# Wider dummy matmuls, a second fold on VectorE in the pairs that issue weights, and one gather moved up

## The reference

```python
batch, n_heads, seq, head_dim = (4, 8, 768, 64)      # chunk = 32, top_k = 6
ub = sum(maximum(q * k_min[chunk], q * k_max[chunk]), -1)   # causal chunks only
sel = the 6 chunks of largest ub, for each query
scores = where(sel & causal, q @ k.T / sqrt(64), -1e9)
attn = exp(scores - max) / (sum(exp(scores - max)) + 1e-09)
x = (attn @ v), heads side by side                   # 3072 tokens x 512
logits = x @ w_gate                                  # 8 experts
expert_idx, gate_w = argmax(logits), its softmax weight
for e in range(8):
    tok_idx = tokens of expert e, the 80 of largest gate_w if there are more
    h = maximum(x[tok_idx] @ w1[e], 0.0)             # 512 -> 1024
    out[tok_idx] = gate_w[tok_idx] * (h @ w2[e])     # 1024 -> 512
```

## Time and profile before

| | us |
|---|---|
| median of 3 runs | 274.03 (273.4 to 276.74) |
| the profiled execution | 270.66 |
| its span, first to last instruction | 268.9 |
| TensorE busy | 258.0 (96%) |
| POOL busy | 216.9 (81%) |
| VectorE busy | 214.0 (80%) |
| ScalarE busy | 149.6 (56%) |

### The profile page before, as it was taken

How to read it: one execution, slowest core, us unless ns; L and a number is a source line. 1 busy time by engine, 2 the same in 40 slices (tenths; PEclk the granted TensorE clock), 3 DMA queues, 4 the chain that set the end, 5 groups by cost and what they waited for, 6 DMA issues and landing times.

```text
span 268.9 us, 9115 instructions
## 1 busy us (share of the span) xinstructions
PE 258.0 (96%) x3812; PEld 164.1 (61%) x3812; DVE 214.0 (80%) x576; ACT 149.6 (56%) x227; POOL 216.9 (81%) x286
## 2 busy tenths in 40 slices
PE   7999999999999999999999999999999998989993
PEld 7456666665656566666655666656565656676663
DVE  6896797687979989777979898999899997983332
ACT  2295656565676564646674546564856564863220
POOL 6067989998999899997999899989999961726862
PEclk9999999999999999999999999999999999999999
DMA  9989999999799979998999899999899896841882
GB/s 149 181 146 151 243 228 275 203 178 224 117 214 170 205 127 195 164 218 142 202 153 214 156 189 157 216 165 311 168 214 258 224 212 161 135 102 39 142 169 77
DMA packets 148616, 48.34 MB, mean 180 GB/s; under 512 B 131583, under 2 KB 138870, under 8 KB 148512
## 3 DMA queue, kind: packets, MB, share of 16 engines
q1 hardware_dynamic: 135504, 28.73, 53.4%
q0 software_dynamic: 9936, 18.64, 38.3%
q10 hardware_dynamic: 3136, 0.39, 0.9%
HBM read 57.03 MB, written 11.01 MB: 253 GB/s over the span
## 4 chain that ended last, share of the span: by engine, by line
PE 62%; POOL 25%; issue 4%; DMA 3%; DVE 3%; ACT 2%; ACTq 1%; POOLq 0%; DVEq 0%
PE OB L632 19%; PE SC L546 19%; POOL ES L600 16%; PE SC L567 4%; POOL EXB L586 4%; PE MM L668 3%; PE MM L474 2%; PE MM L645 2%; PE OB L716 2%; PE OB L1380 2%; DMA qn<-x_rows,idx 1%; DMA qn<-in_q_dram 1%; ACT EXB L576 1%; PE SC L1354 1%; PE MM L513 1%
## 5 line engine op out<-in xcount | busy, mean ns | idle before, releaser
L576 ACT ACTIVATE EXB<-SC 128x1024 f32<-128x1024 f32 (+1 forms) x87 | 83.1, 966 | 36.6 <-PE SC L546 25.0
L600 POOL TENSOR_TENSOR ES<-ES,EXB 128x256 f32<-128x256 f32 (+1 forms) x87 | 91.1, 1048 | 5.6
L546 PE MATMUL SC<-qT,kT 64*128 64x512 f32 (+3 forms) x476 | 86.3, 464 | 0.4 <-ACT EXB L576 0.3
L632 PE MATMUL OB<-EXB,vn 128*64 128x256 f32 (+3 forms) x704 | 73.4, 362 | 0.9 <-POOL EXB L586 0.9
L632 PEld LDWEIGHTS OB<-EXB,vn 128*64 128x64 f32 x704 | 45.9, 137 | 25.7 <-issue 10.4
L546 PEld LDWEIGHTS SC<-qT,kT 64*128 64x128 f32 x476 | 39.2, 187 | 16.5 <-issue 11.0
L600 POOL TENSOR_TENSOR ES<-EXB 128x512 f32<-128x512 f32 (+1 forms) x29 | 45.2, 1559 | 2.4
L586 POOL TENSOR_SCALAR_AFFINE_SELECT EXB<-EXB 128x256 f32<-128x256 f32 x79 | 34.2, 442 | 5.5 <-ACT EXB L576 5.5
L640 ACT ACTIVATE oT<-OB 128x512 f32<-128x512 f32 (+1 forms) x32 | 15.7, 490 | 40.6 <-PE OB L632 40.6
L567 PE MATMUL SC<-unsT,ind 64*128 64x256 bf16 (+5 forms) x238 | 35.6, 295 | 0.1
L567 PEld LDWEIGHTS SC<-unsT,ind 64*128 64x128 bf16 x238 | 11.8, 95 | 15.9 <-issue 6.2
(11 more groups left out here) (269 smaller groups left out, 405.8 us busy)
## 6 DMA issues: line engine op xcount, KB each, us to landing
w1s<-in_moe_w_dram POOLq DMA_DIRECT2D x8, 1024.0 KB, 8.9
w2s<-in_moe_w_dram POOLq DMA_DIRECT2D x7, 1024.0 KB, 13.9
vn<-in_v_dram SPq DMA_DIRECT2D x32, 192.0 KB, 4.4
kn<-in_k_dram SPq DMA_DIRECT2D x62, 96.0 KB, 2.9
qn<-in_q_dram SPq DMA_DIRECT2D x62, 96.0 KB, 3.8
out_dram<-w1s SPq DMA_DIRECT2D x2, 1536.0 KB, 7.0
out_dram<-out_dram SPq DMA_DIRECT2D x2, 1536.0 KB, 9.5
x_rows<-xp SPq DMA_DIRECT2D x7, 384.0 KB, 4.9
```

What stands on the lines that cost most here:

```text
L546: op("pe", lambda: pe.matmul(o, kT[j][pr, ts(kt)], qT[j][pr, q0:q1], start=not flags and (not cols or cols[0] == 0), stop=bool(flags)), r= ...
L576: op("act", lambda: ac.activation(Ex(st, None, 0, W), src, ACTF.Exp, scale=SCALE), r=pk, w=[f"E{st}"])
L600: op(e, lambda: sy.queue[e].tensor_tensor(o, in0, in1, ALU.add), r=[f"E{s2}", f"E{first[0]}"] if first else [f"E{s2}"] + kt, w=kt)
L632: op("pe", lambda: pe.matmul(OB[pr, q0:q1], vn[s][:, kt, h, :], ex, start=(n == 0), stop=last), r=[f"vn{s}{h}", "ES0" if st is None else f ...
```

## The change

1. `warm` issues wide matmuls: one weight load of the identity and up to 4 x 128 columns, the identity read again and again through an access pattern of stride 0. `warm(62)` becomes 15 matmuls of 512 columns and one of 256.
2. `WPLAN` moves ahead of `fold`. In its pairs POOL leaves out (5, 0, 640, 768), and `own_fold` does it on VectorE behind its first addition, on E5 and ES5. Pair 13 is direct and is as before.
3. `turn_next(2)` issues gather 6 behind gathers 4 and 5 and no blocks; `turn_next(3)` issues blocks 0 and 1, `turn_next(4)` gather 7 and blocks 2 and 3, `turn_next(5)` blocks 4 to 7. POOL's order becomes gathers 4, 5 and 6, scatter 0, blocks 0 and 1, scatter 1, gather 7, blocks 2 and 3, blocks 4 to 7, scatter 2.

```diff
+                WPLAN = {2: (0, 1), 4: (2, 3), 6: (4, 5), 8: (6, 7), 10: (8, 9), 12: (10, 11), 13: (12,)}
...
-                    for (s2, c2, q0, q1) in [a for a in ADDS[st] if i in (0, NP - 1) or a != (4, 0, 384, 512) and not (direct(i) and a == (5, 0, 640, 768))]:
+                    for (s2, c2, q0, q1) in [a for a in ADDS[st] if i in (0, NP - 1) or a != (4, 0, 384, 512) and not ((direct(i) or i in WPLAN) and a == (5, 0, 640, 768))]:
...
                         op("dve", lambda: ve.tensor_tensor(o, o, Ex(4, None, 0, 128), ALU.add), r=["E4", "ES3"], w=["ES3"])
+                        if i in WPLAN:
+                            o5 = ES[:, :, 640:768]
+                            op("dve", lambda: ve.tensor_tensor(o5, o5, Ex(5, None, 0, 128), ALU.add), r=["E5", "ES5"], w=["ES5"])
...
                 def warm(n):
-                    for _ in range(n):
-                        op("pe", lambda: pe.matmul(SC[0][:, 0:128], ident_bf[:], ident_bf[:], start=True, stop=True),
+                    for k in range(0, n, 4):
+                        w = min(4, n - k)
+                        op("pe", lambda: pe.matmul(SC[0][:, 0:w * 128], ident_bf[:], bass.AP(ident_bf, 0, [[128, 128], [0, w], [1, 128]]), start=True, stop=True),
                            r=["ident_bf"], w=["SC0"], inc=False)
...
                     if e < 5:
-                        for n in {2: (4, 5), 3: (6,), 4: (7,)}[e]:
+                        for n in {2: (4, 5, 6), 3: (), 4: (7,)}[e]:
                             gather(n, (f"xS{e}",))
-                        last_w2(((0, 1), (2, 3), range(FB // 2, FB))[e - 2])
+                    if 2 < e < 6:
+                        last_w2(((0, 1), (2, 3), range(FB // 2, FB))[e - 3])
```

More of the change, by code:

```diff
@@ L1123, in rank_late @@
                     gate_gcols(bb)
-                WPLAN = {2: (0, 1), 4: (2, 3), 6: (4, 5), 8: (6, 7), 10: (8, 9), 12: (10, 11), 13: (12,)}
                 for i in range(NP):
```

## The result

On the same occasions the kernel before took 273.17 us (median of 22 runs) and the changed kernel 270.42 (median of 22, 269.8 to 273.32): ratio 0.9926, 95% interval 0.9901 to 0.9951, so about 2.0 us by the ratio, where 4.0 were forecast. Ratios here leave out disturbed runs, and the medians do not; so a ratio is not the quotient of the medians beside it.

A forecast was written before the change was run, and what follows sets the result against it. TensorE, busy 258.0 of 268.9 us, bounds the kernel, so only its waits can pay. Gains of 1.0 (part 1), 2.4 (part 2) and 0.65 (part 3) sum to 4.0, taking 274.03 to 270.0 us; range 268.8 to 272.8.

The forecast's parts named there:

- the head: Start of kernel: wide dummies end near 8.0 to 8.5 us, covered by VectorE's work until L474 at 8.63; price 0.
- the hole: Last pair's summing matmuls (L707): a 1.0 us gap from an emptied instruction buffer closes with 92 fewer instructions; gain 1.0.
- Rival 4: Start: the clock rises later, so the first real matmuls run at 1.2 GHz; slower, price taken as 275 us, chance 0.05.
- Rival 1: Last pair's sums (L707): the gap without a releaser stays or moves, so 1.0 us is lost; 271.0 us, chance 0.22.
- what closes counts whole: Behind L707: VectorE waits there and its chain leads to the last gate, so the full 1.0 us is gained.
- Four stretches: Pairs 3, 4, 5 and 9: TensorE's excess over like stretches without weights goes: 0.34, 0.31, 0.88, 0.88, together 2.4 us.
- Rivals 2 and 3: Second fold takes 1.06 us: 272.0 us, chance 0.15; POOL not the cause of TensorE's waits: 272.4 us, chance 0.06.
- rival 2's mechanism: At the second fold, VectorE and POOL get in each other's way, as in POOL's 1.33 against 0.73 us.
- the 0.65: Expert 6's transposes (L1335): gather 6 starts 2.5 us earlier, so TensorE's wait for it goes; gain 0.65 us.
- Gather 7: Expert stage: it arrives at 257.6 where TensorE wants it at about 257.5; loss 0, at worst 0.1 us.
- The blocks that part 3 moves: Expert stage: blocks 0 to 3 move back under 3 us, the last four stay; first used in the last round.
- signs of error: Wrong if L668 waits for the new fold, a new releaserless hole opens, or the first pair's matmuls take twice their time.

The follow-up runs named there:

- e_after2: The changed kernel unaltered, run a third time, on the third chip: 268.03 us, ratio 0.9910 to the kernel before, span 266.2.
- first profile: The first profiled execution of the changed kernel: 270.01 us, span 268.3, against 270.66 and 268.9 for the kernel before.
- e_no3b: Parts 1 and 2 without part 3, run once more on the third chip: 268.91 us, ratio 0.9917 to the kernel before, span 266.2.
- e_pad: The changed kernel plus 46 tiny matmuls behind the wide dummies, restoring TensorE's old instruction count: 269.0 us, ratio 0.9938 to the kernel before.
- e_part1: The kernel before with only part 1, the wide dummies: 269.94 us, ratio 0.9972 to the kernel before.
- e_part2: The kernel before with only part 2, the second fold on VectorE: 267.42 us, ratio 0.9893 to the kernel before.
- e_part3: The kernel before with only part 3, the new order in the expert stage: 271.28 us, ratio 1.0017 to the kernel before.
- e_no1: Parts 2 and 3 with the 62 narrow dummies kept: 274.7 us, ratio 0.9927 to the kernel before.
- e_part2b: Part 2 alone on the kernel before, run once more on the second chip: 273.23 us, ratio 0.9856 to the kernel before.
- e_after: The changed kernel unaltered, run again on the second chip: 273.5 us, ratio 0.9942 to the kernel before, span 271.5.
- e_no3: Parts 1 and 2 without part 3, on the second chip: 270.9 us, ratio 0.9838 to the kernel before.
- e_late_w1: Parts 1 and 2, with the last expert's 1 MB weight block issued behind gathers 2 and 3: 273.19 us, ratio 1.0086 to the kernel before.

## Why the prediction came out as it did

The predicted 270.0 was met by the median of 270.42, partly by luck: the kernel before was at 273.17, not 274.03, on those occasions, and the gain was 1.6 to 2.5 us by the three ratios (0.9942, 0.9926, 0.9910), not 4.0. The execution that answers the sum best is `e_after2`, which has no late copies. Start times of four rows, and the span:

| | before | first profile | `e_after2` | `e_no3b` |
|---|---|---|---|---|
| L645/L650, pair 2 | 38.73 | 38.86 | 38.90 | 38.74 |
| L645/L650, pair 15 | 219.42 | 217.01 | 217.62 | 217.63 |
| L810/L815 | 231.22 | 227.62 | 228.23 | 228.23 |
| first L1354/L1358 | 241.27 | 237.67 | 238.69 | 238.67 |
| span | 268.9 | 268.3 | 266.2 | 266.2 |

Read from `e_after2`: 0.17 lost at the head, 1.97 gained over the pairs, 1.19 at the hole, 0.41 lost at gather 0, 0.12 gained in the expert stage: 2.7 us.

- **Part 1, the head:** right in what counts. VectorE releases L474 in every profile but `e_pad`, at 8.65 to 9.28 us with the wide dummies and 8.60 to 9.01 with the narrow ones, so no price of them shows. The dummies ended at 6.88 to 8.21, mostly earlier than the 8.0 to 8.5 of the prediction: 512 columns take 0.43 us at first and 0.22 later (1.2 and 2.4 GHz), and this step up comes at about 5 us in the first profile and 7.5 in `e_part1`, always ahead of L474. (The granted clock in the earlier trace rows reads 1.00 throughout; the step is read from these distances alone.) Rival 4 is out: L474 and the first scores last as long as before.
- **Part 1, the hole:** the reading held; that a buffer runs empty there is still inferred, but the place is shown. The hole is there in the seven profiles where TensorE has the old number of instructions (both of before, `e_part2`, `e_part3`, `e_pad`, `e_no1`, `e_part2b`; 0.43 to 1.21 us) and at neither place in the seven with 92 fewer. Counted in the trace with its semaphore instructions, TensorE has the same 6,336 or 6,337 instructions ahead of it in all seven. With part 2 there are six semaphore instructions fewer, and the hole stands three matmuls and three weight loads further on, at L727. Rival 1 is out. The Trainium skill (Runtime: NRT & Kernel Launch, Instruction fetch mechanics) calls the crossing of a block boundary mostly hidden; in this run of 128 matmuls and 128 weight loads in 2.6 us the traces disagree.
- **Part 1, what the hole is worth:** the step that failed is "what closes counts whole". Up to L810/L815 it holds: from the last L645/L650 to there it is 10.6 us in all seven profiles without the hole and 11.8 before. Behind that stands gather 0, which waits for the 1 MB block. The issue of the block is released by L707 and so moves with it, but the block lands 8.6 to 10.5 us later. Where it took 9.5 us or more the wait in front of L915 or L920 took back 0.4 (`e_after2`, `e_no3b`) and 0.5 us (`e_part1`); where it took 9.0 or 9.1 (first profile, `e_after`, `e_no3`) nothing was lost. Why it varies is open. And at L727, where the hole stands with part 2, it costs less: holes of 0.52 to 1.21 us make the same stretch 0.2 to 0.9 us longer, at L707 holes of 0.43 to 0.97 made it 0.7 to 1.2 longer. The prediction added the parts as if they were independent.
- **Part 2:** right in every step up to the fold. Four stretches, 2.4 us, and the fold (L611) 2.7 us for six, 0.44 each against the 0.46 taken; L673 never waited for it. Rivals 2 and 3 are out as they stood. But rival 2's mechanism, the two engines in each other's way, came true at an instruction of which the prediction didn't speak. In five of the ten profiles with part 2 TensorE waits 0.5 us at L637 in pair 11 for VectorE's L748. VectorE in `e_after2`, then POOL:

```profile
164.43 1.10 DVE L1024 CAST dTb<-dT 80x40 bf16<-80x40 f32 x1
...
165.53 0.94 DVE L748 TENSOR_TENSOR xp<-OB,rden 128x768 bf16<-128x768 f32 x1
```

```profile
164.23 1.27 POOL L602 TENSOR_TENSOR ES<-ES,EXB 128x512 f32<-128x512 f32 x1
```

and VectorE in the first profile, where POOL's same fold began at 164.21:

```profile
164.12 0.18 DVE L1024 CAST dTb<-dT 80x40 bf16<-80x40 f32 x1
```

The cast of 80 x 40 takes 1.10 us in those five profiles, where it starts 0.20 behind POOL's fold and ends with it, and 0.18 in the other five, where it starts 0.09 to 0.16 ahead. The Trainium skill (SBUF — State Buffer, Who interferes with whom) says that VectorE and GpSimd share a pair of ports that the first holds for its whole instruction while the other stands still, and that a cast can need it; the rows agree. In the kernel before, the cast was 0.15 us ahead of that fold; part 2 makes POOL earlier in this pair, and which comes first then differs from run to run. So part 2 is worth 2.4, or 1.9 where this race is lost.
- **Part 3:** the step that failed is the 0.65 itself. It was read from a wait that stands in both profiles of the kernel before (0.65 and 0.55) but in none of the five of kernels with part 1 or 2 and the old order. The move itself did what was forecast: from expert 2's transposes to gather 6 it is 6.12 us before (244.88 to 251.00) and 3.57 in `e_part3` (246.86 to 250.43), 2.55 earlier against the 2.5 forecast. But nobody wanted it so early. Gather 7, costed at "0, at worst 0.1", makes TensorE wait 0.48 in `e_after2`, but 0.56 with the old order, so that isn't part 3's either. Gather 6 of `e_part1`, issued 0.05 us from its place before (251.00), and the rows that TensorE takes from it without a wait:

```profile
250.95 1.04 POOL L1264 DMA_INDIRECT qn<-x_rows,idx  x1 [0.30 <-issue]
...
254.17 0.32 PE L1336 MATMUL MM<-ident_bf,qn 80*128 80x80 bf16 x4
```

So what differs is the gather's flight: at most 3.2 us here, 3.9 and 3.8 in the two profiles of before. Why it is shorter with parts 1 or 2 is open. On the second chip part 3 was a loss: ratio 0.9942 with it, 0.9838 without (273.5 against 270.9 us); its late copies were the longer ones. The blocks that part 3 moves were put at nothing; `e_pad` and `e_part3` show 0.6 and 0.2 us for them.
- **The rest:** of the signs of error, a new hole without a releaser came only in `e_no3`, 0.29 us at L1358 and 0.23 at L1384, in a profile with late copies. What came besides was a kind of wait that no rival had, the late copies. What sets them is not settled. They go with the chip or the occasion: they are in all four profiles on the second chip and in none of the eight on the first and third, and in two of three profiles of one and the same program. They stand in the stretch in which POOL issues gathers and scatters, and on the second chip they were longer (4.2 us against 1.0 to 1.4) where part 3 puts three gathers and a scatter in a row. What POOL does with them was not tried apart. No profile of the kernel before was taken on that chip, so it isn't shown that it has them too.

Parts 1 and 2 without part 3 were equal to the whole change on the third chip and ahead of it on the second, so that is the version to keep of these two. Part 2 alone is not told apart from it: 0.9856 against 0.9838 on the second chip, with intervals of 0.7% to either side.

## What to carry to other kernels

A wait for a transfer, even one that two profiles show, may go by itself when another part of the change is made, and its time should not be added to theirs: the wait for gather 6 was in both profiles of before and in none with part 1 or 2. The term that rested on four like stretches held best. Before adding up what several edits bring, follow the path behind each to the next transfer in a queue: here a block of 1 MB in front of a small gather took back, in three profiles, a part of what was won ahead of it. A fold moved off GpSimd can cost more than its own time, where another VectorE instruction now meets GpSimd's next one.

## What the runs showed that was not expected

- A hole at a boundary of TensorE's instruction packets lasts 0.43 to 1.21 us in a dense stretch, and 46 matmuls of no use at the head of the program (92 instructions with their weight loads) bring it back in the last pair, some 220 us later.
- A gather behind a block of 1 MB in POOL's queue lands 6.2 to 8.0 us after its issue; with the block behind it (`e_late_w1`), gathers 0 and 1 landed after 3.9 and 2.9 us.
- A wait of TensorE can cost more than its length: behind the 3.80 us of `e_late_w1` the granted clock was 0.50 in 252 to 254, and 32 matmuls of L1357 took 2.33 us in place of 1.31.
- On some occasions ScalarE and VectorE take some of TensorE's results 0.8 to 4.2 us after the matmuls' end in the expert stage, on others VectorE always within 0.05; the cause is open.
